# A two-layer mixture kernel behind a Fourier transform: first group of the second layer at fixed addresses, feature transform from half-width columns, gate parts moved between rounds

## What is computed

```python
def reference(x, moe, moe2):
    a = np.fft.fft(np.fft.fft(x, axis=1), axis=2).real   # x: 4 x 2496 x 256
    h = _moe_ref(a.reshape(9984, 256), **moe)            # 8 experts, 1248 rows each
    return _moe2_ref(h, **moe2)                          # 8 experts, argmax of the gate

# _moe_ref: logits = x @ w_gate; (row, expert) pairs in falling order of logit, a row goes
#   to the first expert with room; out = relu(x @ w1[e]) @ w2[e]
# _moe2_ref: e = argmax(x @ w_gate); out = softmax weight of e * sigmoid(x @ w_output_gate)[e]
#   * relu(x @ w1[e]) @ w2[e]
```

## Time and profile before

| | us |
|---|---|
| median of 3 executions | 1352.18 |
| lowest, highest | 1351.89, 1353.84 |
| the profiled execution, its time | 1355.83 |
| its span in the trace | 1354.1 |
| PE busy | 1277.1 (94%) |
| DVE, ACT, POOL busy | 761.8, 324.8, 520.2 |
| mean granted clock of PE | 0.934 |

### The profile page before, as it was taken

The page is one execution under the profiler, slowest core; times in us unless marked ns, Lnnn a source line. Parts: engine busy times, 40 slices in busy tenths (PEclk is TensorE's granted clock), DMA queues, the critical chain, the costliest instruction groups (busy, mean ns, idle before and its releaser), DMA issues.

```text
span 1354.1 us, 30708 instructions
## 1 busy us (share of the span) xinstructions
PE 1277.1 (94%) x10392; PEld 1175.9 (87%) x10393; DVE 761.8 (56%) x2029; ACT 324.8 (24%) x787; POOL 520.2 (38%) x531
## 2 busy tenths in 40 slices
PE   8998999579999999999999997999999999999996
PEld 5666888558879888889999996999999999999996
DVE  6935888878585678775443544433333334333332
ACT  1013010122322323333232331222222222222221
POOL 0000011226465656555657541612443252544411
PEclk9999555579999999999999998999999999999998
DMA  7717241022212121212222221221232121232110
GB/s 322 269 62 264 91 141 64 1 76 70 83 54 87 58 83 59 75 63 87 61 84 77 68 86 43 87 68 40 78 107 74 43 90 52 77 107 75 47 39 20
DMA packets 63129, 115.98 MB, mean 86 GB/s; under 512 B 7736, under 2 KB 45377, under 8 KB 62912
## 3 DMA queue, kind: packets, MB, share of 16 engines
q1 hardware_dynamic: 39264, 72.16, 15.5%
q0 software_dynamic: 11808, 31.03, 7.0%
q10 hardware_dynamic: 11968, 11.63, 3.2%
HBM read 81.64 MB, written 34.45 MB: 86 GB/s over the span
## 4 chain that ended last, share of the span: by engine, by line
PE 74%; DVE 11%; issue 2%; DMA 1%; ACT 1%; POOL 0%; ACTq 0%; DVEq 0%; POOLq 0%; SPq 0%
PE bank L1105 22%; PE bank L1107 22%; PE bank L1106 21%; PE bank L986 3%; PE bank L969 3%; DVE hot_r L1784 2%; PE bank L1254 1%; PE bank L1117 1%; DVE hot_q L1785 1%; DVE hot_q L1783 1%; DVE hT_low L1954 1%; DVE arena L1663 1%; DVE xT_low L1947 0%; DVE arena L1728 0%; DVE arena L1657 0%
## 5 line engine op out<-in xcount | busy, mean ns | idle before, releaser
L1105 PE MATMUL bank<-weights_high,hT_high 128*128 (+1 forms) x1328 | 388.6, 293 | 0.0
L1107 PE MATMUL bank<-weights_high,hT_low 128*128 (+1 forms) x1328 | 378.4, 285 | 0.0
L1106 PE MATMUL bank<-weights_low,hT_high 128*128 (+1 forms) x1328 | 377.2, 284 | 0.0
L1105 PE MATMUL bank<-xT_high,weights_high 128*128 128x256 f32 (+2 forms) x1072 | 335.2, 313 | 9.2 <-DVE hT_low L1954 3.7
L1107 PE MATMUL bank<-xT_high,weights_low 128*128 128x256 f32 (+2 forms) x1072 | 331.1, 309 | 0.0
L1106 PE MATMUL bank<-xT_low,weights_high 128*128 128x256 f32 (+2 forms) x1072 | 330.4, 308 | 0.0
L1106 PEld LDWEIGHTS bank<-weights_low,hT_high 128*128 128x128 f32 x1328 | 250.4, 189 | 0.0
L1105 PEld LDWEIGHTS bank<-weights_high,hT_high 128*128 128x128 f32 x1328 | 250.2, 188 | 0.1
L1107 PEld LDWEIGHTS bank<-weights_high,hT_low 128*128 128x128 f32 x1328 | 250.2, 188 | 0.0
L1105 PEld LDWEIGHTS bank<-xT_high,weights_high 128*128 128x128 f32 x1072 | 204.6, 191 | 24.5 <-DVE hT_low L1954 7.8
L1107 PEld LDWEIGHTS bank<-xT_high,weights_low 128*128 128x128 f32 x1072 | 203.9, 190 | 11.3
(11 more groups left out here) (264 smaller groups left out, 1404.4 us busy)
## 6 DMA issues: line engine op xcount, KB each, us to landing
arena<-middle ACTq DMA_DIRECT2D x44, 258.0 KB
spectrum<-arena SPq DMA_DIRECT2D x39, 256.0 KB, 2.2
arena<-in_w2a_t SPq DMA_DIRECT2D x8, 1024.0 KB, 4.8
raw<-in_w1a SPq DMA_DIRECT2D x8, 1024.0 KB
raw<-in_w2a SPq DMA_DIRECT2D x8, 1024.0 KB
raw<-in_w1b SPq DMA_DIRECT2D x8, 1024.0 KB
raw<-in_w2b SPq DMA_DIRECT2D x8, 1024.0 KB
arena<-in_x SPq DMA_DIRECT2D x4, 768.0 KB, 4.4
```

What stands on the lines that cost most here:

```text
L1105: pe.matmul(out_, a[0], b[0], start=start, stop=False)
L1106: pe.matmul(out_, a[0], b[1], start=False, stop=False)
L1107: return pe.matmul(out_, a[1], b[0], start=False, stop=stop)
```

## The change

1. *Feature stage.* The sine half goes through PE apart from the cosine half, with 129 columns each (`LC` = 129, `RC` = 137). `seqB` meets `feat_s` of 2 x 137 columns: in the first 137 only the alternating row, in the other 137 only the sines. `seqA` meets `feat_c` of 137 columns, added to the first 137. ACT copies the first half (`cosines`) to one of three buffers `cosine`, and both halves' logits to `both`. DVE adds and subtracts the halves (`pairs`), which gives columns 0 to 128 of the row and of the mirrored row. ACT makes the other 127 columns of both by copying `store` mirrored (`mirrored`). Both engines work on every tile. The logits' sums and differences come in three pieces (`pair_logits`). SP's four small stores stand together behind tile 33.
2. *Gate parts.* A table, `GATE_PARTS`, gives how many stand behind each round.
3. *Second layer.* Its first group has its rows at address 0 and expert 0's slot as constants; `list_tables` takes at least one group for that expert. SP loads the rows (`first_rows`) when the first group of the last expert is scattered and, if fewer than 256 rows of that kind were counted by then (`late_i`), the rest too. PE transposes and multiplies ahead of `m2.row`, the tables' semaphore; DVE splits the transposed rows ahead of the tables; ACT does three of the four hidden quarters ahead of its wait for them. The spins change from 24 behind the counts to 9 ahead of the places. `result2(0)` is split around `x_turn2(1)`.

```diff
+LC = D // 2 + 1
+RC = LC + E
...
+COSINES = 3
...
+GATE_PARTS = [0, 0, 2, 2, 5] + 3 * [2, 2, 2, 2, 5] + [2, 2, 2, 2, 8]
...
-SPIN_START, SPIN_LISTS, SPIN_TURN, SPIN_TABLES, SPIN_BRANCH = 24, 12, 2, 24, 4
+SPIN_START, SPIN_LISTS, SPIN_TURN, SPIN_KINDS, SPIN_BRANCH = 24, 12, 2, 9, 4
...
             for n in range(NB + 1):
-                sp.wait_ge(s_out[n % 2], n // 2 + 1)
+                sp.wait_ge(s_out, n + 1)
...
-                for b in range(B):
-                    if g == max(b * HALF // P, LAST_AT):
+                if n == BOUND_STEPS[0] + 4:
+                    sp.wait_ge(s_bound, 2)
+                    for b in range(B):
...
+            def first_rows(done):
+
+                sp.dma_start(xg_all, middle[0:W2, :].rearrange("(j p) r -> p j r", p=P)).then_inc(done, 16)
+
+            sp.wait_ge(m1.place, E * NG - NG + 1)
+            sp.sem_inc(s_hold, 1)
+            late = sp.value_load(late_i[0:1, 0:1], min_val=0, max_val=1)
+            sp.wait_ge(m1.sent[0], 16 * TILES[0] * E)
+            for gi in range(1, NG):
+                sp.wait_ge(m1.sent[gi], late * (16 * TILES[gi]) + 16 * TILES[gi] * (E - 1))
+            first_rows(m2.got)
...
                 if n >= 4:
-                    pe.wait_ge(s_out[n % 2], n // 2 - 1)
+                    pe.wait_ge(s_paired, n - 3)
...
-                pe.matmul(bk[0:m, 0:RC], a, feat_c[:], start=True, stop=False)
-                pe.matmul(bk[0:m, 0:RC], s, feat_s[:], start=False, stop=True).then_inc(s_f_ps, 1)
+                    at_ = slice(g * P, (g + 1) * P)
+                    pe.matmul(bk[:].rearrange("p (h c) -> p h c", h=2)[:, :, 0:RC], seqB[:, at_], feat_s[:],
+                              start=True, stop=False)
+                    pe.matmul(bk[:, 0:RC], seqA[:, at_], feat_c[:], start=False, stop=True).then_inc(s_f_ps, 1)
...
+            def cosines(n):
+
+                act.wait_ge(s_f_ps, n + 1)
...
+                if n >= COSINES:
+                    act.wait_ge(s_paired, n - COSINES + 1)
+                act.copy(cosine[:, n % COSINES], bk[:, 0:LC])
+                act.copy(both[:, :, rows_at(n)], bk[:].rearrange("p (h c) -> p h c", h=2)[:, :, LC:RC]).then_inc(s_cosine, 1)
+
+            def mirrored(n):
+
+                act.wait_ge(s_paired, n + 1)
...
+                u = rows_at(n) % NST
+                act.copy(store[:, u, :, LC:D], store[:, u, ::-1, P - 1:0:-1]).then_inc(s_out, 1)
+
+            for n in range(NB + 1):
+                cosines(n)
+                if n:
+                    mirrored(n - 1)
+            mirrored(NB)
...
+            def pairs(n):
+
+                dve.wait_ge(s_cosine, n + 1)
...
+                if g >= NST:
+                    dve.wait_ge(s_stored[g % NST], 16 * (g // NST))
+                c, t = cosine[:, n % COSINES], feature_bank(n)[:, D:D + LC]
+                dve.tensor_tensor(store[:, g % NST, 0, 0:LC], c, t, ALU.add)
+                dve.tensor_tensor(store[:, g % NST, 1, 0:LC], c, t, ALU.subtract).then_inc(s_paired, 1)
...
+            for n in range(NB + 1):
+                pairs(n)
                 if n == BOUND_AT:
+                    pair_logits(0, BOUND_AT)
                     bound(0)
+                if n == BOUND_STEPS[0] + 2:
+                    pair_logits(BOUND_AT, n)
...
+                        elif fast:
+                            pe.wait_ge(m1.h, E * NG * FCH + 3)
+                            pe.wait_ge(m1.split, (E + 1) * SPLITS)
+                            spin(SPIN_KINDS)
...
+            x_turn2(0)
+            spin(SPIN_BRANCH)
+            pe.wait_ge(m2.xT, 2 * GP)
+            hidden_from(0, E % 2)
             pe.wait_ge(m2.row, 1)
             pe.sem_inc(s_hold, 1)
             last = pe.value_load(last_i[0:1, 0:1], min_val=MIN2 - 1, max_val=G2 - 1)
-            x_turn2(0)
-            hidden2(0)
-            with pe.Fori(0, last) as i:
+            result2(0, E % 2, [0])
+            x_turn2(1)
+            result2(0, E % 2, [1])
+            hidden2(1)
+            with pe.Fori(1, last) as i:
...
+            x_out2(0)
+            h_out2(0, 0, HB - 1)
             for gi in range(NG):
                 act.wait_ge(m1.sent[gi], 16 * TILES[gi] * E)
+            act.wait_ge(m2.gt, GP)
             act.wait_ge(m2.row, 1)
             act.sem_inc(s_hold, 1)
+            load2(1)
             last = act.value_load(last_i[0:1, 0:1], min_val=MIN2 - 1, max_val=G2 - 1)
...
+            h_out2(0, HB - 1)
```

More of the change, by code:

```diff
@@ L163, in constants @@
     d = np.arange(P)[:, None]
[L164 to L170, removed]
+    l = np.arange(D)[None, :]
+    fc, fs = np.cos(2 * np.pi * ((d * l) % D) / D), -np.sin(2 * np.pi * ((d * l) % D) / D)
+    put("feat_c", fc[:, 0:LC])
+    alternate = (-1.0) ** np.arange(LC)[None, :] * (d == 0)
+    put("feat_s", np.concatenate([alternate, fs[:, 0:LC]], 1))
+    fs[0] = (-1.0) ** np.arange(D)
+    put("featT_c", np.concatenate([fc[:, h * P:(h + 1) * P].T for h in range(2)], 1))
+    put("featT_s", np.concatenate([fs[:, h * P:(h + 1) * P].T for h in range(2)], 1))
     put("ident", np.eye(P))
@@ L180, in constants @@
     p = np.arange(P)[:, None]
-    put("sign", np.where(np.arange(P) == 0, 1.0, -1.0)[:, None])
+    put("inner", np.stack([np.arange(P) == 0, np.arange(P) > 0], 1))
     put("lane", p)
@@ L663, in _ @@
                 sp.wait_ge(again.raw, (E + 1) * 32 + 32)
+                for gi in range(NG):
+                    sp.wait_ge(again.sent[gi], 16 * TILES[gi] * E)
+                sp.wait_ge(m2.got, 16)
+                first_rows(again.raw)
+                sp.wait_ge(again.raw, (E + 1) * 32 + 48)
                 sp.sem_inc(s_hold, 1)
@@ L1163, in places @@
                         route_read(m.place, e * NG + gi + 1)
+                    if first_count:
+                        pe.matmul(bank[7][:, w * E:w * E + E], ones_b[:], kinds_up[gi][:, :, w], start=True, stop=True)
                     pe.matmul(to, tri_b[:], kinds_in[gi][:, :, 1:1 + w].rearrange("p e k -> p k e"), start=True, stop=False)
@@ L1444, in x_out2, with h_out2 @@
                              bank[j][:, 0:D].rearrange("p (c n) -> p c n", c=DCH)).then_inc(m2.xT_high, 1)
-            def h_out2(i):
-                for q in range(HB):
+            def h_out2(i, first=0, stop=HB):
+                for q in range(first, stop):
                     act.wait_ge(m2.h_ps, i * HB + (q + 1))
@@ L1593, in bound @@
                 if part == 0:
-                    for u in range(2):
-                        dve.wait_ge(s_out[u], BOUND_AT // 2 + u)
                     dve.memset(ones_f[:], 1.0)
@@ L1627, in _ @@
                         bound(part + 1)
-            for u in range(2):
-                dve.wait_ge(s_out[u], NB // 2 + 1)
+            pair_logits(BOUND_STEPS[0] + 2, NB)
             dve.wait_ge(s_llast, 16 * B)
@@ L2043, in expert @@
                             gated(e, gi)
-                        placed(e, gi)
+                        placed(e, gi, fast and last and gi == 0)
                 return x_out, h_out, expert
@@ L2051, in _ @@
             dve.sem_inc(m1.h, 3)
+            dve.sem_inc(m2.xT, GP)
+            dve.sem_inc(m2.h, HB - 1)
             name(on_limit.link, open_log)
@@ L2222, in _ @@
                 slow_expert(E - 1, 1, True)
-                list_tables(slow.link, 2, again.tables)
+                dve.wait_ge(s_list, 2)
+                dve.memset(same_f[:, 0:1], 0.0).then_inc(again.tables, 1)
                 dve.wait_ge(again.tables, 1)
```

138 lines of the change are left out of this document (68 added, 70 removed).

## The result

| | us | ratio to before, 95% interval |
|---|---|---|
| before, median of 5 | 1352.18 | |
| changed, median of 5 | 1345.10 | 0.9941, 0.9930 to 0.9951 |
| changed again, 5 runs | 1343.47 | 0.9933, 0.9920 to 0.9947 |
| changed a third time, 6 runs | 1345.49 | 0.9942, 0.9929 to 0.9955 |
| predicted | 1333.9 | range 1330.0 to 1341.0 |

The kernel became faster by 0.6 to 0.7%, some 8 us, where 18.3 were predicted. The time lies outside the range, on its slow side.

The account below looks back on a forecast made before the run. PE was 74% of the chain of waits, its columns bounding the feature stage, with PE idle between the stages. Terms 7.0 - 0.5 + 11.8 = 18.3 us off the median of 1352.18 gave 1333.9 us, range 1330 to 1341.

Parts of the forecast that it names:

- The branches: Between the stages, the branch on the flag was to cost PE 0.53 us and DVE 0.7, bounds 0.4 and 1.4.
- the 1.3 us of waiting for the tables: In the second layer's first group, PE was to wait 1.3 us for DVE's tables before its second half.
- the term of 11.8: Between the stages, the second group's first matmul was to come 11.8 us earlier, bounds 9 and 12.5.
- PE's clock in the new first group: Rival, 12%: PE's clock falls there, 48 matmuls at 0.217 us each, total time 1337 to 1339 us.
- The feature stage: Stage before routing: fewer PE columns and a shorter tail were to gain 7.0 us, bounds 3 and 10.
- The tile: Feature stage: a tile of 411 columns in place of 546 was to take PE 0.69 us, not 0.92.
- ACT keeps up: Feature stage: ACT's three copies were to take 0.54 us a tile, by interpolation from earlier copies.
- the first rival: Feature stage, 12%: ACT's copies do not overlap, a tile takes 0.84 us, total time 1337.4 us.
- The stores: Feature stage: stores were to reach 345 GB/s, 0.76 us a tile, slower than PE's 0.69.
- From the first tile to tile 33: Feature stage: this stretch was to take 25.3 us in place of 31.4, with 1.5 of new stalls.
- The tail: From tile 33 to routing's first operation: 6.9 us in place of 7.8, a gain of 0.9.
- The gate parts: Routing phases: moving the parts was to lose 0.5 us together, bounds 0 and 1.5.

Follow-up runs that it names:

- all_first: Changed kernel with the second layer's first-group work on PE, ACT and DVE ahead of the jump over the slow path: 1340.05 us, then 1340.68.
- gates_undone: Changed kernel with the gate parts put back where they stood before the change: 1346.84 us.
- pe_first: Changed kernel with only PE's transposes and first hidden part ahead of its jump, ACT and DVE jumping where they did: 1344.27 us.

## Why the prediction was wrong

**The branches: the step that failed.** "The branch on the flag takes 0.53 us" and for DVE "I take 0.7, bounds 0.4 and 1.4". The jump over the slow path cost PE 4.40 us and, in the next block, 2.41; DVE 3.72 and ACT 2.98 where each could be seen. The row that gave 0.53 stood behind 24 spins of 5.83 us, which the change itself took away from that place. The prediction saw that DVE's branch "was hidden behind other waits", and took its price from a row that was half hidden too. It put the first hidden product 3.1 us behind the counts; it was 9.73, and 9.73 to 10.26 in all six profiles that have this order: 6.6 us too early. From there to the second group it had 13.3 us, and 13.13 were measured; there the size fits in part by luck, since the 1.3 us of waiting for the tables were 0.22 and the products longer instead. Of the term of 11.8, 5.4 came, or 5.2 by the means of the profiles (28.44 to 23.24), below its lower bound of 9.

None of the rivals was this one. The Trainium skill's rule cited above spoke against this very part of the change, and the prediction didn't weigh it.

**PE's clock in the new first group.** This rival (12%) came true in part: the clock was at 0.50 from about 817 to 824, after PE had stood for 4.4 us. But the 48 products took 6.3 us, not 10.4, since it rose after the first few, and they ended at 829.2 where DVE's tables, the next thing PE needed, ended at 828.4. In the two other profiles of the changed kernel they took 7.1 and 6.9 us, and the way to the second group stayed 13.1. So this clock cost next to nothing here. In all_first, with no such gap, it stayed at 1.00 during these products in both profiles (6.0 us); in the second it fell behind them, from 821.7 to 825.1.

**The feature stage: mechanism right, size near.** Predicted gain 7.0, bounds 3 and 10; measured 6.06, and 4.9 to 6.9 in the 13 profiles that have it. Step by step:
- The tile: 0.69 predicted, 0.69 measured.
- ACT keeps up by the interpolation from the earlier trace rows, 0.54 us a tile; where it catches up, it takes 0.55 (113.58 to 114.13):

```profile
113.58 0.40 ACT L1368 COPY arena<-arena 128x254 f32<-128x254 f32 x1
113.89 0.26 ACT L1358 COPY arena<-bank 128x129 f32<-128x129 f32 x1
114.05 0.18 ACT L1359 COPY arena<-bank 128x16 f32<-128x16 f32 x1
114.13 0.40 ACT L1368 COPY arena<-arena 128x254 f32<-128x254 f32 x1
```

  The estimate of 0.81 us from the fixed costs that the Trainium skill gives for ScalarE ("VectorE: DVE Perf Modes", "The TRN2 errata") was wrong here, and with it the first rival. By themselves the three took 0.40, 0.26 and 0.18 us, about what these figures give (0.40, 0.25, 0.16); but each starts before the one ahead of it has ended, so their sum isn't the pace.
- The stores: 345 GB/s estimated, 333 measured at a share of 0.99. DVE waited for them by 0.61 us at tile 9 and by 0.68 and 0.66 at tiles 23 and 24, and its additions at tile 25 joined in; PE kept to 0.69 us a tile from tile 6 to tile 27.
- From the first tile to tile 33: 25.3 us predicted, 25.9 measured. The new stalls were 2.1 us in place of 1.5.
- The tail, predicted 6.9 us: 7.2 here. Routing waits for the four small stores in 6 of the 13 profiles, by 1.0 to 1.5 us, and in the 7 others for nothing; so they land about when routing could start, as it was put.

**The gate parts: mechanism right.** Predicted 0.5 us lost; the prefix came 125.71 us behind routing's start, against 125.13 and 125.37 before: 0.3 to 0.6 lost. The prediction let the wait for the load grow by some 5 us without the move; gates_undone shows 4.27 us in place of 0.60, 3.7 more, and 3.4 us of the time. The direction held, the size was less.

**Not in the prediction:** 0.8 us in the second layer's groups, in every kernel with the feature stage, cause open.

In sum: 6 from the features, 0.4 lost to the parts, 5.2 between the stages, 0.8 lost in the groups make 10; the three comparisons gave 7.1 to 9.9, with the executions themselves 2 to 3 us apart.

## What to carry to other kernels

An idle time that stands behind filler work is what is left of a cost, not its price: ask what the filler covered before taking the filler away. A jump over a large piece of code loads its target from memory, some 3 to 4.5 us an engine here with the read of the flag and more for the next block, but the load runs while the engine works through what is queued; put such a jump where the engine has queued work and then waits anyway, or let the likely code run straight on ahead of it. Loads of several engines run side by side, so moving one of them alone may give nothing; and look at the clock behind each new wait.

## What the runs showed of the hardware

- A taken jump over the slow path, the read of the flag included: 4.40 to 4.77 us on PE and 2.41 to 2.86 more some way into the code behind it, 3.72 and 3.88 on DVE, 2.98 and 3.21 on ACT. The read with no jump behind it takes PE 1.07 us (all_first, pe_first). With PE's jump go two loads of about 16 KB on the queue q8; PE goes on some 1.5 us behind each landing. Behind 24 queued matmuls nothing of it is to be seen. For DVE and ACT no run takes the jump out: DVE's idle time moves along with its jump (3.36 us in all_first), and that ACT's is such a load is argued, not shown.
- The granted clock can fall for some 3 us in one execution and not in the next of the same kernel (288 to 291 us, 2 of 16 profiles), at a cost of 1.6 us there.
- ACT's three short copies of a tile, two out of PSUM and one out of SBUF, overlap to 0.55 us for 399 columns.
